# Folding one weight product into the next: four quarters in place of two halves, and the last weight sets split one step later

## The reference

```
h = x @ w_in;  g = max(0.01 * h, h);  y = g @ w_out           # 512 -> 2048 -> 512
a = y @ w1;  b = y @ w2;  z = ((a * b) @ w3) @ w_out2           # 512 -> 1024 -> 1024 -> 512
```

## Time and profile before

| | us |
|---|---|
| median of 3 runs | 535.73 (534.71 to 536.19) |
| the profiled execution, its own time | 534.71 |
| its span | 532.9 |
| PE busy | 527.1 |
| DVE, ACT, POOL busy | 266.5, 172.5, 93.8 |

### The profile page before, as it was taken

The page is one execution under the profiler, slowest core; times in us unless marked ns, Lnnn a source line. Parts: engine busy times, 40 slices in busy tenths (PEclk is TensorE's granted clock), DMA queues, the critical chain, the costliest instruction groups (busy, mean ns, idle before and its releaser), DMA issues.

```text
span 532.9 us, 9081 instructions
## 1 busy us (share of the span) xinstructions
PE 527.1 (99%) x3652; PEld 432.2 (81%) x3652; DVE 266.5 (50%) x387; ACT 172.5 (32%) x299; POOL 93.8 (18%) x89
## 2 busy tenths in 40 slices
PE   8999999999999999999999999999999999999997
PEld 6888877777788888888888888888888888888885
DVE  5757365676533322222424678586777744322322
ACT  5443323233333221222323235542222214332221
POOL 2232221213000000000002993222222200000000
PEclk9999999999999999999999999999999999999999
DMA  8998563432230000000001111012111111105002
GB/s 300 337 396 281 191 240 119 140 119 82 81 98 20 1 0 1 0 1 0 1 0 41 39 60 59 2 39 62 58 41 39 39 41 38 42 2 196 1 1 79
DMA packets 22344, 43.85 MB, mean 82 GB/s; under 512 B 3344, under 2 KB 3352, under 8 KB 22304
## 3 DMA queue, kind: packets, MB, share of 16 engines
q1 hardware_dynamic: 19824, 35.66, 19.7%
q10 hardware_dynamic: 2448, 7.62, 4.2%
q0 software_dynamic: 32, 0.00, 0.0%
HBM read 38.03 MB, written 5.25 MB: 81 GB/s over the span
## 4 chain that ended last, share of the span: by engine, by line
PE 99%; issue 0%; ACT 0%; DVE 0%; DVEq 0%
PE acc L969 14%; PE acc L971 13%; PE acc L970 13%; PE hid L969 13%; PE hid L971 12%; PE hid L970 12%; PE hid L1188 5%; PE hid L1187 5%; PE hid L1186 5%; PE hid L1000 1%; PE hid L1027 1%; PE hid L1014 1%; PE hid L1038 1%; PE hid L1060 1%; PE acc L1038 0%; PE acc L1027 0%
## 5 line engine op out<-in xcount | busy, mean ns | idle before, releaser
L969 PE MATMUL acc<-g_hi,wb 128*128 128x512 f32 x286 | 112.1, 392 | 0.0
L970 PE MATMUL acc<-g_lo,wb 128*128 128x512 f32 x286 | 111.4, 390 | 0.0
L971 PE MATMUL acc<-g_hi,wb 128*128 128x512 f32 x286 | 111.3, 389 | 0.0
L969 PE MATMUL hid<-xy_hi,wa_hi 128*128 128x512 f32 x256 | 100.5, 393 | 0.0
L970 PE MATMUL hid<-xy_lo,wa_hi 128*128 128x512 f32 x256 | 99.7, 390 | 0.0
L971 PE MATMUL hid<-xy_hi,wa_lo 128*128 128x512 f32 x256 | 99.6, 389 | 0.0
L822 DVE TENSOR_TENSOR g<-g,hid 128x512 f32<-128x512 f32 (+1 forms) x48 | 33.0, 687 | 97.3 <-ACT g L618 97.1
L618 ACT ACTIVATE g<-hid 128x512 f32<-128x512 f32 (+1 forms) x48 | 28.7, 598 | 135.6 <-PE hid L971 135.6
L750 DVE TENSOR_TENSOR g_lo<-g,g_hi 128x512 fp32r<-128x512 f32 (+1 forms) x64 | 51.1, 798 | 39.7 <-ACT g_hi L624 32.9
L969 PEld LDWEIGHTS acc<-g_hi,wb 128*128 128x128 f32 x286 | 53.7, 188 | 11.4
L971 PEld LDWEIGHTS acc<-g_hi,wb 128*128 128x128 f32 x286 | 53.7, 188 | 11.2
(11 more groups left out here) (135 smaller groups left out, 640.7 us busy)
## 6 DMA issues: line engine op xcount, KB each, us to landing
stage<-weights SPq DMA_DIRECT2D x88, 256.0 KB, 3.4
w_out_place<-attn ACTq DMA_DIRECT2D x12, 512.0 KB, 4.9
outT<-x_hi_place SPq DMA_DIRECT2D x11, 256.0 KB, 3.3
x_hi_place<-attn SPq DMA_DIRECT2D x4, 512.0 KB, 7.9
w_out_place<-attn SPq DMA_DIRECT2D x4, 512.0 KB, 8.3
w_dram<-x_lo_place SPq DMA_DIRECT2D x8, 256.0 KB, 6.1
stage<-w_dram SPq DMA_DIRECT2D x8, 256.0 KB, 2.8
x_lo_place<-attn SPq DMA_DIRECT2D x2, 512.0 KB, 6.1
```

The costliest lines, as they stand in the source:

```text
L969: nc.tensor.matmul(out, w_hi, a_hi, start=first, stop=False)
L970: nc.tensor.matmul(out, w_hi, a_lo, start=False, stop=False)
L971: return nc.tensor.matmul(out, w_lo, a_hi, start=False, stop=final)
```

## The change

The 64 products come in four quarters of two blocks (QUARTER = 2) in place of two halves of four. A tile w3 still holds four products, which are now two steps k of two blocks. The quarters take turns in the banks: hid[:, 0] for the even ones, acc[:, 0:2] for the odd. ACT copies two blocks behind each quarter, three times ahead of a w3 tile and once at the end. The first step is two products, and products 2 and 3 stand ahead of the spreads (POW_AFTER = 4), so these still follow four products. SP loads nine tiles ahead of load_part(0, 0) in place of eight, and three in place of two between it and load_part(0, 1). EARLY_34 follows from the order: 15 tiles in place of 14. Last, set 2 of "again" is no longer split at f = 3 of the stretch before; sets 2 to 7 stand at f = 1 to 6 of the last loop, as set f + 1. The order of the matmuls and their number are otherwise the same.

```diff
-HALF = 4
-N34 = F2 * K34 // HALF
+QUARTER = 2
+N34 = F2 * K34 // 4
+POW_AFTER = 4
-SPLIT_AGAIN = (1, 3)
-PRODUCTS = [(part, k, slot) for part in range(F2 // HALF) for k in range(K34) for slot in range(HALF)]
+PRODUCTS = [(quarter, k, slot) for quarter in range(F2 // QUARTER) for k in range(K34) for slot in range(QUARTER)]
@@ w34_tiles
-        if slot == 0:
-            tiles += [("w3", i // HALF)] + [("wl", k)] * (part == 0)
+        tiles += [("w3", i // 4)] * (i % 4 == 0) + [("wl", k)] * (quarter == 0 and slot == 0)
-COPY_BEFORE = [("w3", K34 + RING34 - 1), ("out", W_OUT_AHEAD)]
+COPY_BEFORE = [("w3", 4 * quarter + RING34 + 3) for quarter in range(3)] + [("out", W_OUT_AHEAD)]
-        w34_acc = [hid[:, 0, 0, :], hid[:, 0, 1, :], acc[:, 0, :], acc[:, 1, :]]
+        def w34_acc(quarter):
+            banks = hid[:, 0] if quarter % 2 == 0 else acc[:, 0:QUARTER]
+            return [banks[:, slot, :] for slot in range(QUARTER)]
@@ SP
-            for w in range(8):
+            for w in range(9):
                 load_weight(w)
             load_part(0, 0)
-            for w in range(8, 10):
+            for w in range(9, 12):
                 load_weight(w)
             load_part(0, 1)
-            for w in range(10, 12):
-                load_weight(w)
@@ ACT, and the same on DVE with weight_lo
-                if f in SPLIT_AGAIN:
+                if f == 1:
                     for _ in range(2):
                         weight_hi(w)
                         w += 1
...
                 copy_gate(f)
                 round_gated(N1 + 2 * F2 + f, gate_ready, f, g[:, f % 2, :])
-                if f + 2 < F2:
+                if f + 1 < F2:
                     for _ in range(2):
                         weight_hi(w)
                         w += 1
@@ PE, w34_products
-                    if part > 0 and k == 0:
-                        pe.wait_ge(w34_copied, slot + 1)
+                    if quarter > 1 and k == 0:
+                        pe.wait_ge(w34_copied, QUARTER * (quarter - 2) + slot + 1)
@@ PE, start
-            first_step = [slice(slot * P, (slot + 1) * P) for slot in range(HALF)]
+            first_step = [slice(slot * P, (slot + 1) * P) for slot in range(QUARTER)]
...
+            w34_products(QUARTER, POW_AFTER)
...
-            w34_products(HALF, first_product(1))
+            w34_products(POW_AFTER, first_product(1))
```

More of the change, by code:

```diff
@@ L109, in w34_tiles @@
     for i in range(begin, end):
-        part, k, slot = PRODUCTS[i]
-        if slot == 0:
-            tiles += [("w3", i // HALF)] + [("wl", k)] * (part == 0)
+        quarter, k, slot = PRODUCTS[i]
+        tiles += [("w3", i // 4)] * (i % 4 == 0) + [("wl", k)] * (quarter == 0 and slot == 0)
     return tiles
@@ L405, in load_weight, with store_w34 @@
                     store_w34(COPY_BEFORE.index(ORDER[w - STAGE]))
-            def store_w34(part):
-                for f in range(HALF * part, HALF * (part + 1)):
+            def store_w34(quarter):
+                for f in range(QUARTER * quarter, QUARTER * (quarter + 1)):
                     wait_then_step(w34_copied, f + 1)
@@ L542, in place_is_free @@
                 if kind == "w3" and i >= RING34:
-                    act.wait_ge(w34_done, HALF * (i - RING34 + 1))
+                    act.wait_ge(w34_done, 4 * (i - RING34 + 1))
                 if kind == "out":
                     if i < K34:
-                        act.wait_ge(w34_done, len(PRODUCTS) - HALF * (K34 - i - 1))
+                        act.wait_ge(w34_done, len(PRODUCTS) - QUARTER * (K34 - i - 1))
                     elif i < 10:
-                        act.wait_ge(w34_done, len(PRODUCTS) - HALF * (K34 + RING34 - i - 1))
+                        act.wait_ge(w34_done, len(PRODUCTS) - 4 * (K34 + RING34 - i - 1))
                     else:
@@ L570, in weight_hi, with copy_w34 @@
                 nc.scalar.copy(hi, staged_tile(w, hi)).then_inc(hi_done, 1)
-            def copy_w34(part):
-                for slot in range(HALF):
-                    f = HALF * part + slot
+            def copy_w34(quarter):
+                for slot in range(QUARTER):
+                    f = QUARTER * quarter + slot
                     if f >= KD_TILES:
                         act.wait_ge(w34_stored, 16 * (f - KD_TILES + 1))
-                    act.wait_ge(w34_done, HALF * K34 * (part + 1) - HALF + slot + 1)
-                    nc.scalar.copy(w34_copy(f), w34_acc[slot]).then_inc(w34_copied, 1)
+                    act.wait_ge(w34_done, QUARTER * K34 * (quarter + 1) - QUARTER + slot + 1)
+                    nc.scalar.copy(w34_copy(f), w34_acc(quarter)[slot]).then_inc(w34_copied, 1)
             def x_hi(c):
@@ L601, in _ @@
                 for tile in segment_order(s):
-                    if tile == COPY_BEFORE[0]:
-                        copy_w34(0)
+                    if tile in COPY_BEFORE:
+                        copy_w34(COPY_BEFORE.index(tile))
                     weight_hi(w)
@@ L609, in _ @@
             x_hi(EARLY_CHUNKS - 1)
-            copy_w34(1)
+            copy_w34(3)
             load_after(EARLY_CHUNKS - 1)
@@ L975, in w34_products @@
                 for i in range(begin, end):
-                    part, k, slot = PRODUCTS[i]
-                    w3_hi, w3_lo = w3(i // HALF)
+                    quarter, k, slot = PRODUCTS[i]
+                    w3_hi, w3_lo = w3(i // 4)
                     for tile in w34_tiles(i, i + 1):
                         pe.wait_ge(split_done, CREDIT_SPLIT + PLACE[tile] + 1)
-                    if part > 0 and k == 0:
-                        pe.wait_ge(w34_copied, slot + 1)
-                    cols = slice(slot * P, (slot + 1) * P)
-                    last = product(w34_acc[slot], w3_hi[:, cols], w3_lo[:, cols], *wl(k),
+                    if quarter > 1 and k == 0:
+                        pe.wait_ge(w34_copied, QUARTER * (quarter - 2) + slot + 1)
+                    cols = slice(i % 4 * P, (i % 4 + 1) * P)
+                    last = product(w34_acc(quarter)[slot], w3_hi[:, cols], w3_lo[:, cols], *wl(k),
                                    k == 0, k == K34 - 1)
@@ L1060, in _ @@
                 nc.tensor.matmul(hid[:, 0, 0, 0:2 * P], probs[:, 0, 0:2, :], probs[:, 0, :, :], start=True, stop=True)
-            first_step = [slice(slot * P, (slot + 1) * P) for slot in range(HALF)]
+            first_step = [slice(slot * P, (slot + 1) * P) for slot in range(QUARTER)]
             pe.wait_ge(hi_done, max(PLACE["w3", 0], PLACE["wl", 0]) + 1)
             for slot, cols in enumerate(first_step):
-                nc.tensor.matmul(w34_acc[slot], w3(0)[0][:, cols], wl(0)[0], start=True, stop=False)
+                nc.tensor.matmul(w34_acc(0)[slot], w3(0)[0][:, cols], wl(0)[0], start=True, stop=False)
             pe.wait_ge(split_done, CREDIT_SPLIT + PLACE["w3", 0] + 1)
             for slot, cols in enumerate(first_step):
-                nc.tensor.matmul(w34_acc[slot], w3(0)[1][:, cols], wl(0)[0], start=False, stop=False)
+                nc.tensor.matmul(w34_acc(0)[slot], w3(0)[1][:, cols], wl(0)[0], start=False, stop=False)
             pe.wait_ge(split_done, CREDIT_SPLIT + PLACE["wl", 0] + 1)
             for slot, cols in enumerate(first_step):
-                nc.tensor.matmul(w34_acc[slot], w3(0)[0][:, cols], wl(0)[1], start=False,
+                nc.tensor.matmul(w34_acc(0)[slot], w3(0)[0][:, cols], wl(0)[1], start=False,
                                  stop=False).then_inc(w34_done, 1)
+            w34_products(QUARTER, POW_AFTER)
             pe.wait_ge(selector_loaded, 16)
@@ L1132, in _ @@
             pe.wait_ge(x_split, CREDIT_X + EARLY_CHUNKS)
-            pe.wait_ge(w34_copied, HALF + 2)
+            pe.wait_ge(w34_copied, 3 * QUARTER)
             hidden(0, 0, 0)
@@ L1303 @@
     w3_blocks = np.asarray(moe2_w3).reshape(F2, P, K34, P)
-    w3_t = np.stack([w3_blocks[HALF * part + slot, :, k].T for part, k, slot in PRODUCTS])
-    w3_t = w3_t.reshape(N34, HALF, P, P).transpose(0, 2, 1, 3).reshape(N34, P, TOK)
+    w3_t = np.stack([w3_blocks[QUARTER * quarter + slot, :, k].T for quarter, k, slot in PRODUCTS])
+    w3_t = w3_t.reshape(N34, 4, P, P).transpose(0, 2, 1, 3).reshape(N34, P, TOK)
     w_last = moe2_w_out.reshape(K34, P, TOK)
```

## The result

| | before | after |
|---|---|---|
| median of 4 runs each, us | 535.61 | 541.68 (541.51 to 543.2) |
| the profiled execution, us | 534.71 | 541.92 |
| its span, us | 532.9 | 540.1 |

What follows compares the result with a forecast made beforehand. It took PE, busy 527.1 of 532.9 us, as the bound. Adding 5.64 (last loop) and 0.41 (front) gave 540.76 from the profiled execution and 541.78 from the median; it forecast 541.3, range 539.7 to 543.4 us.

Steps and rivals of the forecast that it cites:

- PE has no idle time, so a late tile is paid in full and nothing can be won: Whole kernel: PE busy 527.1 of 532.9 us, one 1.5 us wait; removed waits give nothing back, lateness beyond slack costs fully.
- The last loop, 0.94 for a set, six sets, 5.64: Gates 2 to 7 in the last loop: each waits for its set's first tile, 0.94 us each, 5.64 in all.
- where I took 0.06: Last loop: 0.06 us assumed from the end of DVE's lo to PE's start.
- The 0.11 for starting from a stop: Last loop: after idle, PE's second matmul comes 0.34 us behind the first, not 0.23, adding 0.11 per stop.
- What the chain is: Last loop: the tile's lo stands behind copy, multiply, cast and lo, 3.29 us against 2.52 until PE asks.
- rival 2: At gate(f + 1): first tile ready within 12 matmuls if the chain shrinks by 0.8; no wait, 535.1 us; chance 0.05.
- gate(1) and the output stores: Last loop: gate(1) untouched; first two blocks' stores move some 8 us plus two waits, ending well ahead of the end.
- The front, 0.41 at product 16: First 20 us: tile 12 lands at 17.7, its lo is ready at 19.12, so product 16 starts 0.41 us late.
- for which I had found 0.15: Products 2 and 3, seventh in the matmuls, wait for tile 2's lo: 0.15 us late, counted inside the 0.41.
- The sign named for the front: Profile after, near 18.8 us: one PE wait for wb of about 0.4 us.
- The sum: Whole kernel: 5.64 + 0.41 gives 540.76 from the profiled execution, 541.78 from the median; the middle, 541.3, is forecast.
- The clock: Last loop: granted clock stays full; a rival had stops sending PE to 1.2 GHz, 33 us more, 574; chance 0.01.

Runs made afterwards that it cites:

- e2_front: The changed kernel with sets 2 to 7 of "again" put back where they were before, so the quarters alone; 535.56 us, ratio 1.0001.
- e1: The kernel before with the late sets alone: sets 2 to 7 of "again" split at f = 1 to 6 of the last loop; 541.52 us, ratio 1.0109.
- e7: The changed kernel with the set's casts right behind ACT's copy and its lo parts right behind DVE's multiply; 535.44 us, ratio 1.0005.
- e5: The kernel before with sets 2, 3, 4 split late in the last loop and 5, 6, 7 a step ahead; 538.32 us, ratio 1.0056.
- e3: The changed kernel with DVE taking the lo of the set's tiles ahead of the lo of the gated result; 541.41 us, ratio 1.0104.
- e6_cast_first: The changed kernel with ACT casting the set's tiles right behind its copy, ahead of the gated result's cast; 542.36 us, ratio 1.0130.
- e8: The quarters alone with POW_AFTER = 2, the spreads of the powers ahead of products 2 and 3; 535.08 us, ratio 0.9997.
- e4: The changed kernel with set f + 1 split ahead of the step's copy, multiply, cast and lo on ACT and DVE; 535.81 us, ratio 1.0000.

## Why the prediction was right

1. *PE has no idle time, so a late tile is paid in full and nothing can be won.* Right: the quarters alone are within -0.5 to +0.6 us of before, though ACT's copies, the stores and the loads all lie elsewhere, and in the profile of e2_front the 1.10 us that PE was late at product 16 (19.87 against 18.77) are still there at the first copy of the last loop (476.11 against 475.01).
2. *The last loop, 0.94 for a set, six sets, 5.64.* Right in mechanism, number of waits and place, and shown by e1 (alone), e7 (its cause taken away inside the step) and e5 (half the number, half the cost). The size was 1.04, 6.2 in all. Nearly all of the 0.10 is the start: from the end of DVE's lo (479.25) to PE's first matmul (479.39) it is 0.14, where I took 0.06. The 0.11 for starting from a stop was read from a row that does not show one: the spreads' last matmul runs until 9.36 and PE's list has no wait there, so the matmul at 9.29 in the earlier trace rows did not start from idle. The same holds for the start of product 16 at 18.77. That the loop's stops then cost nearly the same, 0.12, is luck.
3. *What the chain is.* I wrote that the tile stands behind the copy, the multiply, the cast and the lo, and that rival 2 decides once this chain shrinks by 0.8. The length was right, and e7 bears the rule out: with the chain shortened to 1.91 there is no wait. But e3 showed that taking the lo out of it does next to nothing. The rows had it: the two casts run from 476.88 to 478.02, so the first ends at about 477.5, and its lo begins at 477.61.
4. *gate(1) and the output stores.* Right: gate(1) has no wait, and SP begins the stores of the first two output blocks at 489.57 in place of 479.43, with 50 us to go.
5. *The front, 0.41 at product 16.* Wrong in place. Tile 12 landed 3.8 us after its issue, not 4.3, and its lo was in time. In the quarters' kernel whose front was as early as that of before (e6_cast_first) PE began product 16 at 18.77, the same as before. What was late was tile 2, for which I had found 0.15. It landed at 5.2 in the trace of before, and I took that for a fixed time. The sign named for the front, a wait for wb near 18.8, was in no profile. The other tiles landed where the prediction had them: 10 and 11 at 13.0 and 13.7, where it said 12.9 and 13.6.
6. *Tile 2.* Its cast began, in the seven kernels with the quarters, at 6.15, 6.17, 5.84, 5.95, 5.04, 5.72 and 5.84, and in the three with the order of before at 5.23, 6.13 and 5.11. SP issues the first tiles alike in all, so I read this as a spread between executions; why it is wide was not tried. The quarters need the tile for their seventh matmul, the kernel before only for its thirteenth, and there the spreads stand ahead of it as well. In the quarters' kernels with POW_AFTER = 4 the wait for wb follows the cast: 0.7, 0.7, 0.7, 0.5 and 0.2 us for 6.15, 6.17, 5.84, 5.95 and 5.72, none for 5.04; in the kernels with the order of before there is none, at 6.13 either. Score(0) began at 18.8, 18.8, 18.5, 18.6, 17.7 and 18.3 with the quarters (e8 left out), 18.45 in the mean, and at 17.7, 18.3 and 17.5 without, 17.8 in the mean: a difference of 0.6, but the two groups overlap, and three and six single executions do not show it. The times do not either: the four kernels with the quarters and no wait in the loop (e2, e4, e7, e8) are -0.04, +0.21, +0.44 and +0.08 us from the median of before, 0.17 in the mean. What the front costs is open between nothing and some 0.6, and no run shows the term of 0.41.
7. *The sum.* The forecast added 5.64 + 0.41 = 6.05, and the medians are 6.07 apart. That they agree this well is luck: the loop's term was 0.6 too small (6.2 measured), and the front's 0.41, which no run shows, made up for most of it.
8. *The clock.* The granted clock was 1.00 throughout the loop and the step 9.20, which is 8.16 and the 1.04 of the stop. The Trainium skill, in "TensorE: Matmul & The Clock Gate", section "A second HAM failure mode: psum-queue depth-cycling", tells of a kernel that lost throughput because short idle stretches made the clock swing; this case's trace does not show that, with a stop of about 1 us in each 9.2. Whether longer stops would bring it on was not tried.

## What to carry to other kernels

Where one engine never waits, ask of each moved preparation what stands ahead of it in the order of the engines that do it, and when the last of that is released; the distance in steps says little. When two engines hand a chain back and forth, measure both paths before shortening one: here neither move alone brought anything and both together brought everything. Look also at what a wait asks for: gate(f) waits for the lo of its tile, but its first two matmuls read only the hi (479.39 and 479.70 in the rows of after; ACT had it at about 478.4). A wait in front of the third matmul alone would let PE begin at about 478.5 and stop for some 0.45 us in place of 0.91; that is an estimate from these rows and was not tried. A landing time early in a kernel is a spread, not a number; give a step that hangs on it a margin of about 1 us, or put independent work behind it.

## What was not expected of the hardware

- After the waits for wa_lo, PE's first matmul came 0.14 to 0.15 us behind the end of DVE's instruction (479.25 to 479.39; in e3_lo_first 479.04 to 479.19), but 0.06 behind it at the wait for wb (7.49 to 7.55). The cause is open.
- The third 256 KB transfer of the program was ready for its cast anywhere from 5.04 to 6.17 us in ten profiled executions, while the first was ready between 3.3 and 3.6.
